# A second softplus whose 1 + u lives in PSUM, three bank pairs instead of four, and two smaller edits in a fused attention and feed-forward kernel

## What is computed

```python
scores = scale * q @ k_p.T            # attention over keys and values averaged by 8
x = softmax(scores) @ v_p             # -> x: 2304 tokens x 512
h = x @ w_in                          # first layer: 512 -> 2048
g = where(h >= 1, h, where(h <= -1, 0, (h + 1)**2 / 4))
x = g @ w_out                         # 2048 -> 512
h = x @ w2_in                         # second layer, the same sizes
g = maximum(h, 0) + log1p(exp(-abs(h)))
out = g @ w2_out
```

## Time and profile before

| | us |
|---|---|
| median of 3 runs | 862.84 |
| lowest and highest | 862.07 and 867.12 |
| the profiled execution | 862.46 |
| its span in the trace | 860.7 |

### The profile page before, as it was taken

The page is one execution under the profiler, slowest core; times in us unless marked ns, Lnnn a source line. Parts: engine busy times, 40 slices in busy tenths (PEclk is TensorE's granted clock), DMA queues, the critical chain, the costliest instruction groups (busy, mean ns, idle before and its releaser), DMA issues.

```text
span 860.7 us, 13035 instructions
## 1 busy us (share of the span) xinstructions
PE 845.8 (98%) x5198; PEld 822.7 (96%) x5198; DVE 592.0 (69%) x618; ACT 490.5 (57%) x700; POOL 360.8 (42%) x290
## 2 busy tenths in 40 slices
PE   8989999999999999999999999999999899999998
PEld 7768999999999999999999999999999899999998
DVE  4983855532233598768657698898899989778642
ACT  3875665644445453444435868978887654445442
POOL 6994677744454600000000498888766500000000
PEclk9979999999999999999999999999999999999999
DMA  8952767565555896454633235675655698645532
GB/s 195 209 126 78 209 209 230 185 220 188 181 183 188 274 395 224 167 220 154 227 109 99 96 123 189 211 243 182 211 200 176 204 397 306 239 164 203 200 113 73
DMA packets 106539, 167.82 MB, mean 195 GB/s; under 512 B 21872, under 2 KB 94448, under 8 KB 101872
## 3 DMA queue, kind: packets, MB, share of 16 engines
q1 hardware_dynamic: 93800, 157.86, 54.9%
q10 hardware_dynamic: 12680, 9.14, 3.7%
HBM read 96.21 MB, written 70.78 MB: 194 GB/s over the span
## 4 chain that ended last, share of the span: by engine, by line
PE 84%; DVE 6%; ACT 3%; DMA 3%; SPq 1%; issue 1%; POOL 1%; ACTq 0%; DVEq 0%
PE ps L1263 41%; PE ps L1281 37%; DVE t_a L1052 2%; DMA ops<-gops 2%; PE ps L1178 1%; DVE ops L1064 1%; PE ps L1215 1%; DMA w_raw<-in_moe_w_in_dram 1%; PE ps L1296 1%; PE ps L1321 1%; PE ps L1199 1%; DVE xs L992 1%; ACT qT L652 1%; PE ps L1155 1%; DVE t_a L1055 1%
## 5 line engine op out<-in xcount | busy, mean ns | idle before, releaser
L1263 PE MATMUL ps<-xs,W 128*128 128x384 f32 x2304 | 408.2, 336 | 0.8 <-DVE ops L1044 0.8
L1263 PEld LDWEIGHTS ps<-xs,W 128*128 128x128 f32 x2304 | 399.3, 188 | 5.8 <-issue 4.9
L1281 PE MATMUL ps<-xs,Tm 128*128 128x384 f32 x1968 | 345.9, 336 | 3.4 <-DVE xs L992 3.0
L1281 PEld LDWEIGHTS ps<-xs,Tm 128*128 128x128 f32 x1968 | 342.2, 189 | 4.3 <-issue 3.5
L744 ACT ACTIVATE xs<-ops 128x768 fp32r<-128x768 f32 (+1 forms) x148 | 111.7, 826 | 159.1 <-PE ps L1281 149.9
L608 POOL TENSOR_TENSOR ops<-ops 128x384 f32<-128x384 f32 x48 | 72.9, 1519 | 303.2 <-DVE ops L1064 221.9
L992 DVE TENSOR_TENSOR xs<-ops,xs 128x768 fp32r<-128x768 f32 (+1 forms) x148 | 130.2, 941 | 1.8 <-ACT xs L744 1.8
L1044 DVE SCALAR_TENSOR_TENSOR ops<-ps,t_a 128x768 f32<-128x768 f32 x48 | 45.9, 956 | 110.4 <-ACT t_a L768 110.2
L766 ACT ACTIVATE t_a<-ps 128x768 f32<-128x768 f32 x48 | 39.0, 812 | 96.2 <-PE ps L1263 96.2
L1077 DVE TENSOR_TENSOR X<-ps,X 128x768 f32<-128x768 f32 x41 | 38.7, 955 | 77.8 <-PE ps L1281 77.8
L1064 DVE TENSOR_TENSOR ops<-t_a,t_b 128x768 f32<-128x768 f32 x48 | 62.8, 1308 | 19.7 <-ACT t_b L787 17.9
(11 more groups left out here) (88 smaller groups left out, 650.6 us busy)
## 6 DMA issues: line engine op xcount, KB each, us to landing
gops<-ops SPq DMA_DIRECT2D x48, 1344.0 KB, 5.8
ops<-gops SPq DMA_DIRECT2D x36, 1536.0 KB, 6.8
X<-gops SPq DMA_DIRECT2D x22, 384.0 KB, 6.4
w_raw<-in_moe_w_in_dram SPq DMA_DIRECT2D x32, 256.0 KB, 3.9
t_raw<-in_moe_w_out_dram SPq DMA_DIRECT2D x6, 1024.0 KB, 10.0
out_dram<-y_out ACTq DMA_DIRECT2D x11, 384.0 KB, 2.6
k_raw<-in_k_dram SPq DMA_DIRECT2D x10, 288.0 KB
q_raw<-in_q_dram SPq DMA_DIRECT2D x20, 144.0 KB, 7.6
```

The costliest lines, as they stand in the source:

```text
L1263: last = mm(banks[:, tb, :], W[:, slot, f, part, c * P:(c + 1) * P], x[:, x_part, at:at + TB], start=c == 0 and s == 0, stop=c == KC - 1 a ...
L1281: last = mm(banks[:, d, :], Tm[:, t, part, j, d * P:(d + 1) * P], g[:, g_part, at * TB:(at + 1) * TB], start=at == 0 and s == 0, stop=at = ...
```

## The change

The softplus becomes: ScalarE |h| and u as before; b = 1 + u goes into the fourth pair of PSUM banks, of which there is one copy; l = ln b from there into one half of t_b. VectorE: s = max(h, 0) + u into the other half of t_b, as soon as u is there; e = (b - 1) - l, read from and written to the b banks; g = s - e. The sum is the same, in another order. Each b waits until the g of the pair before has been made, since that reads the b banks; s waits for the same g. ScalarE does the logarithm of a pair directly behind its 1 + u. The h pairs of the second layer go round three bank pairs, and line 1263 of pair a waits for s of pair a - 3. Step 3 of the second layer's products is the first to use the fourth pair again and waits for the last g.

The first product of each layer was copied to two blocks of X and is now copied to one; the addition that read the other copy reads this one. The hand-written places of fill 4 are gone from the second layer's end, which gets the plain order. SyncE issues the load of the fourth step's operand (fill 6) in quad 22 and no longer in quad 23, ahead of the store of quad 22.

```diff
-Y_OPS = (((0, 0, None), (0, 1, None)), ((0, 0, (0, 0)),), ((0, 1, (0, 1)),), ((1, 0, (0, 1)),),
+Y_OPS = (((0, 1, None),), ((0, 0, (0, 1)),), ((0, 1, (0, 1)),), ((1, 0, (0, 1)),),
+V_PAIRS, V_STEPS = HPAIRS + STEPS, 2 * HPAIRS + STEPS
+        def pair_of(v):
+            if v < SHARED:
+                return SHARED_BANKS[v % 2]
+            if v < V_PAIRS:
+                return ALL_BANKS[(v - SHARED) % 4]
+            if v < V_STEPS:
+                return ALL_BANKS[(V_PAIRS - SHARED + (v - V_PAIRS) % 3) % 4]
+            return ALL_BANKS[(V_PAIRS - SHARED + v - V_STEPS) % 4]
+        def b_banks():
+            b = 2 * ALL_BANKS[(V_PAIRS - SHARED + 3) % 4]
+            return ps[:, b:b + 2, 0:TB]
@@ banks_free
-            return spent[v - 2 if v < SHARED else v - 4]
+            if v == V_STEPS + 3:
+                return g_made, 2 * HPAIRS
+            if v < SHARED:
+                return spent[v - 2]
+            return spent[v - 3 if V_PAIRS + 3 <= v < V_STEPS + 3 else v - 4]
@@ sync
-                    if k == QUADS - 1:
+                    if k == QUADS - 2:
                         load_ops(layer, NT)
@@ scalar: plus_one, log
-                nc.scalar.activation(t_b[:, a % 2, :, :], t_a[:, a % 2, :, :], ACT.Copy, bias=1.0).then_inc(b_made, 1)
+                if a == 0:
+                    act.wait_ge(y_added, y_count(0, STEPS - 1))
+                else:
+                    act.wait_ge(g_made, HPAIRS + a)
+                nc.scalar.activation(b_banks(), t_a[:, a % 2, :, :], ACT.Copy, bias=1.0).then_inc(b_made, 1)
-                act.wait_ge(r_made, a + 1)
-                nc.scalar.activation(t_b[:, a % 2, :, :], t_b[:, a % 2, :, :], ACT.Ln).then_inc(l_made, 1)
+                act.wait_ge(b_made, a + 1)
+                nc.scalar.activation(t_b[:, 0, :, :], b_banks(), ACT.Ln).then_inc(l_made, 1)
@@ scalar: the loop
-                            if a == HPAIRS - 2:
-                                for piece in range(PIECES // 2):
-                                    fill_hi_piece(fill_of(1, NT + 1), piece)
                             exp_abs(a)
-                            if 0 < a < HPAIRS - 1:
-                                log(a - 1)
                             plus_one(a)
-                            if a == HPAIRS - 2:
-                                for piece in range(PIECES // 2, PIECES):
-                                    fill_hi_piece(fill_of(1, NT + 1), piece)
-                                log(a)
+                            log(a)
-                    if layer < m < STEPS:
+                    if m < STEPS:
@@ vector: softplus, total
-                u, b = t_a[:, a % 2, :, :], t_b[:, a % 2, :, :]
-                dve.wait_ge(b_made, a + 1)
-                nc.vector.scalar_tensor_tensor(out=u, in0=b, scalar=1.0, in1=u, op0=ALU.subtract, op1=ALU.subtract
-                                               ).then_inc(r_made, 1)
-                dve.wait_ge(r_made, a + 1)
-                nc.vector.scalar_tensor_tensor(out=u, in0=bank_pair(v_of_pair[n]), scalar=0.0, in1=u,
-                                               op0=ALU.max, op1=ALU.subtract).then_inc(s_made, 1)
+                if a:
+                    dve.wait_ge(g_made, HPAIRS + a)
+                dve.wait_ge(u_made, a + 1)
+                nc.vector.scalar_tensor_tensor(out=t_b[:, 1, :, :], in0=bank_pair(v_of_pair[HPAIRS + a]), scalar=0.0,
+                                               in1=t_a[:, a % 2, :, :], op0=ALU.max, op1=ALU.add).then_inc(s_made, 1)
+                dve.wait_ge(l_made, a + 1)
+                nc.vector.scalar_tensor_tensor(out=b_banks(), in0=b_banks(), scalar=1.0, in1=t_b[:, 0, :, :],
+                                               op0=ALU.subtract, op1=ALU.subtract).then_inc(e_made, 1)
                 dve.wait_ge(s_made, a + 1)
-                dve.wait_ge(l_made, a + 1)
+                dve.wait_ge(e_made, a + 1)
                 dve.wait_ge(*slot_free(u))
-                nc.vector.tensor_tensor(g, t_a[:, a % 2, :, :], t_b[:, a % 2, :, :], ALU.add).then_inc(g_made, 1)
+                nc.vector.tensor_tensor(g, t_b[:, 1, :, :], b_banks(), ALU.subtract).then_inc(g_made, 1)
@@ vector: the loop
                             softplus(a)
-                            if a == HPAIRS - 3:
-                                for piece in range(PIECES // 2):
-                                    fill_lo_piece(fill_of(1, NT + 1), piece)
                             total(a)
-                            if a == HPAIRS - 2:
-                                for piece in range(PIECES // 2, PIECES):
-                                    fill_lo_piece(fill_of(1, NT + 1), piece)
-                    if layer < m < STEPS:
+                    if m < STEPS:
```

More of the change, by code:

```diff
@@ L222, in build @@
         h_abs, u_made, b_made = sem("h_abs"), sem("u_made"), sem("b_made")
-        r_made, s_made, l_made = sem("r_made"), sem("s_made"), sem("l_made")
+        s_made, l_made, e_made = sem("s_made"), sem("l_made"), sem("e_made")
         g_made, s_added = sem("g_made"), sem("s_added")
@@ L247, in wait @@
                 eng.wait_ge(semaphore, value)
+        def pair_of(v):
[6 more added lines that the diff above has]
+            return ALL_BANKS[(V_PAIRS - SHARED + v - V_STEPS) % 4]
         def bank_pair(v):
-            b = 2 * (SHARED_BANKS[v % 2] if v < SHARED else ALL_BANKS[(v - SHARED) % 4])
+            b = 2 * pair_of(v)
+            return ps[:, b:b + 2, 0:TB]
+        def b_banks():
+            b = 2 * ALL_BANKS[(V_PAIRS - SHARED + 3) % 4]
             return ps[:, b:b + 2, 0:TB]
@@ L870, in _ @@
                         fill_hi_piece(fill_of(layer, NT), k - FIRST_AT)
-                if layer == 1:
-                    log(HPAIRS - 1)
                 for m in range(1, STEPS + 2):
-                    if layer < m < STEPS:
+                    if m < STEPS:
                         for piece in range(PIECES):
@@ L1047, in softplus @@
             def softplus(a):
-                n = HPAIRS + a
-                u, b = t_a[:, a % 2, :, :], t_b[:, a % 2, :, :]
-                dve.wait_ge(b_made, a + 1)
-                nc.vector.scalar_tensor_tensor(out=u, in0=b, scalar=1.0, in1=u, op0=ALU.subtract, op1=ALU.subtract
-                                               ).then_inc(r_made, 1)
-                dve.wait_ge(r_made, a + 1)
-                nc.vector.scalar_tensor_tensor(out=u, in0=bank_pair(v_of_pair[n]), scalar=0.0, in1=u,
-                                               op0=ALU.max, op1=ALU.subtract).then_inc(s_made, 1)
+                if a:
[3 more added lines that the diff above has]
+                                               in1=t_a[:, a % 2, :, :], op0=ALU.max, op1=ALU.add).then_inc(s_made, 1)
             def total(a):
                 u, g = g_of(HPAIRS + a)
+                dve.wait_ge(l_made, a + 1)
+                nc.vector.scalar_tensor_tensor(out=b_banks(), in0=b_banks(), scalar=1.0, in1=t_b[:, 0, :, :],
+                                               op0=ALU.subtract, op1=ALU.subtract).then_inc(e_made, 1)
                 dve.wait_ge(s_made, a + 1)
-                dve.wait_ge(l_made, a + 1)
+                dve.wait_ge(e_made, a + 1)
                 dve.wait_ge(*slot_free(u))
-                nc.vector.tensor_tensor(g, t_a[:, a % 2, :, :], t_b[:, a % 2, :, :], ALU.add).then_inc(g_made, 1)
+                nc.vector.tensor_tensor(g, t_b[:, 1, :, :], b_banks(), ALU.subtract).then_inc(g_made, 1)
             def add_y(layer, m):
```

## The result

| | before | after |
|---|---|---|
| median of 20 runs, us | 865.93 | 861.21 |
| lowest | 862.0 | 856.38 |
| profiled execution | 862.46 | 857.14 |
| its span | 860.7 | 855.3 |

The ratio of the runs after to the runs before is **0.994, with a 95% interval from 0.992 to 0.996** (a few runs of each kernel that lie far above the others are left out): 0.6% faster, less than the 1% that the prediction took as the border of "the same". The forecast for the profiled execution was 857.3, and it took 857.14; 862.84 x 0.994 is 857.7, the forecast of the median.

What follows compares the result with a forecast made beforehand. TensorE, with work 98% of the span, was taken as the bound, losing 5.7 us behind the second h stage. 47.40 becomes 41.70 + 0.4 + 0.1 = 42.2, 5.2 us less: 857.3 profiled, median 857.7 us, range 855.8 to 867.

Steps and rivals of the forecast that it cites:

- one verdict: Whole kernel: within 1% of before, chance 0.89; faster by over 1% 0.02, slower by over 1% 0.09.
- The loss before: End of the second h stage through the fifth step: 47.40 us where 41.70 are needed, 5.7 us lost.
- The cause: Second h stage: VectorE's two operations with both inputs in SBUF are blocked by GpSimd's sums, 3.80 us a pair.
- The unknown cost of writing PSUM: Three instructions using b in PSUM: excess zero; bounds 0.1 us less each and, above, one stream doubled, 0.96 to 1.76.
- The ring: Second-layer softplus, serial through the one b buffer (1 + u, ln, e, g, next 1 + u): 3.81 us against TensorE's 4.17.
- The lag of pair 44: Quad 21 of the second h stage: VectorE's weights push s of pair 44 to 6.96 us after its matmuls.
- the last g: End of the second h stage: g of pair 47 done 7.76 us after the last pair's matmuls end.
- The rival's price: Second h stage, softplus chain becomes the bound: full doubling 883 us, chance over 871 0.09; middle 862 to 870, 0.11 shared.
- break-even of 0.3 us: Softplus chain through b: an excess of 0.3 us a pair would eat the 5.7 us of gain.
- rival (2): End of the second h stage stays late by another cause, smaller gain: 858.9 to 862.5 us, chance 0.20.
- Three pairs: Second-layer h pairs on three bank pairs: 5.5 us in reserve, so TensorE shouldn't wait in the h stage.
- The plain order: Fill 4 behind the second h stage: new wait of 0.3 to 0.5 us before the second step; 2.05 us wait goes.

Runs made afterwards that it cites:

- experiment 4: Kernel before with GpSimd's four sums per second-layer quad cut to 8 of 384 columns; ratio to before 0.9912; second h stage's start to first output transpose 241.29 us.
- experiment 6: Changed kernel with the single b buffer in SBUF in place of PSUM, all else as changed; ratio to the kernel before 1.0146.
- experiment 5: Kernel before, old softplus kept, with only its second-layer h pairs going round three bank pairs; ratio to the kernel before 1.0117.
- experiment 3: Changed kernel with the first product copied twice and the load of fill 6 in quad 23 again; ratio to the kernel before 0.9922.
- experiment 8: Changed kernel with 1 + u of each pair done twice over all columns, one behind the other; ratio to the kernel before 1.0279.
- experiment 2: Kernel before with its old softplus and all the other edits of the change; ratio to the kernel before 1.0003.
- experiment 7: Changed kernel with 1 + u of 16 of the 768 columns first and the full one behind a wait for it; ratio to the kernel before 0.9945.

## Why the prediction was right

**What the time alone says.** Little: the range of 855.8 to 867 also holds the 862.84 of no change, and 0.89 of the chances stood on one verdict. The forecast is tested by the places and terms below.

**The loss before.** 5.7 us were counted behind the stage and 5.2 of them forecast as won; 5.6 were won in S to M, of 6.05 that experiment 4's 241.29 leaves to win. The cause, blocked two-input SBUF operations, was argued from three rows; experiment 4 shows it by taking the sums away, and experiment 6 by putting b back into SBUF.

**The unknown cost of writing PSUM.** I took an excess of zero from the nearest rows; it was 0.01 us on VectorE and below zero on ScalarE. With the surcharge for a PSUM source that the Trainium skill's table gives ("VectorE: DVE Perf Modes", the TRN2 errata) the ring would be 3.94 us, an estimate from that table, and the verdict the same. It measured 3.80. The step from e to g did come out 0.07 longer than forecast (1.06), but with b in SBUF it is 1.05 (experiment 6, 630.27 to 631.32), so the trace doesn't show the surcharge.

**The ring.** 3.81 forecast, 3.80 measured. That the sum is right to 0.01 is partly luck: ln to e was 0.07 shorter and e to g 0.07 longer than the distances that I had taken from the old softplus. The lag of pair 44 was 6.7 for 6.96, the last g T + 7.5 for T + 7.76, both 0.3 us earlier than forecast. The rival's price was right where it was tried: 0.85 us more give 1.0279, where the prediction's rule (0.49 x 48 and 5 at the end, less 5.7, that is 22.8 us) gives 1.026. Its break-even of 0.3 us was not tried; at 0.2 the kernel is still 4.3 us faster than before from S to M, where rival (2) expected a gain of 1 to 2 us: the wait was 1.49 us and not 2.4, and no low clock came.

**Three pairs.** They are enough, as forecast, but this was the term that I understood least: experiment 5's 8.7 us against the 4 to 6 expected show how fast a lag turns into waits once cover is short.

**The plain order.** Its new wait was forecast at 0.3 to 0.5 us. The profile shows 0.17 idle behind the modelled end of the first step, and 0.34 more than 48 matmuls from that step's start to the next (668.34 to 677.00), so the size is right. The edit is worth 1.5 us with the new softplus and costs 2.3 us with the old (with the two small edits beside it).

**Copies and load.** Costed at nothing, worth nothing (experiment 3).

**The time itself.** 857.7 was right as a ratio. As a number it was tied to the median of three runs; the twenty runs put both kernels 3 to 4 us higher.

## What to carry to other kernels

Where GpSimd and VectorE both work on SBUF, look for VectorE instructions whose mean is far above their minimum, and move one of their two inputs to PSUM: three instructions for three, and 3.8 us a pair became 2.9. Before a serial ring through one buffer is accepted, add its four start-to-start distances from the trace and hold them against the pace of the bounding engine; 0.36 us of room was enough here; a ring 0.34 us too long on average (experiment 6) or 0.49 us too long (experiment 8) cost all the gain and more. A hand-written order serves one set of durations: when they change, try the plain one again.

## What the runs showed that I had not expected

**Where the scatter comes from.** The second h stage begins at 468.36 us in the profile of before and at 476.97 in that of experiment 2, though the two programs are the same up to 300 us. Pieces of the two chains in order of time, first before, then experiment 2:

```profile
17.90 1.24 PE ps L1178 x20
...
189.60 104.20 PE ps L1263 x600
```

```profile
17.61 2.14 PE ps L1165 x20
...
25.30 1.24 PE ps L1165 x20
...
198.21 104.20 PE ps L1250 x600
```

The third group of this kind starts 7.4 us later in experiment 2 (25.30 against 17.90), the 600 matmuls 8.6 us later. So most of the difference arises in the first 25 us, where 20 matmuls that take 1.24 us elsewhere take 2.14 (17.61), nearly twice as long. Two windows of experiment 2:

```profile
10.00:20.00 10.00, 10.00 (x67) 9.51 (x68) 2.99 (x6) 1.95 (x5) 8.03 (x9) 1.00 0.96 214
60.00:65.00 5.00, 5.00 (x35) 3.91 (x35) 2.77 (x7) 3.16 (x8) 3.77 (x4) 0.50 1.06 223
```

The view prints a clock of 1.00 for the first window. At 61.65 us, where it prints 0.50, the same group of 20 takes 2.21 us again. So it was probably the low clock at the start as well, and the view does not show it; that is inferred from the durations. In all ten profiles the second h stage begins 278.8 us behind the start of the 600 matmuls, whatever the variant, and that start lies anywhere from 189.5 to 198.1 us. A difference of a few us between two profiles of this kernel thus says nothing unless it is counted from S on. Of the twenty runs after, the seven with a mean clock of 0.984 to 0.988 took 861.5 to 864.2 us, the four with 0.994 to 0.996 took 856.4 to 858.0, which fits this.

**A wait and the clock.** After a wait the clock did not always fall, and the length of the wait alone doesn't tell when. Behind 1.41 and 1.66 us (experiment 6) and 1.49 us (experiment 7) it stayed at 1.00. Behind 2.05 us (before), 2.42 (experiment 6), 2.43 and 3.19 (experiment 8) and 4.95 (experiment 2) TensorE ran at 0.50 for a while, which cost 1.5 to 2.2 us. But in experiment 5 the clock stayed at 1.00 behind waits of 2.17 and 2.35 us and fell behind one of 2.40, and in experiment 8 it stayed behind one of 2.40 (682.03). Experiment 5, behind 2.35 and behind 2.40 us:

```profile
676.00:680.20 4.20, 4.20 (x24) 4.20 (x25) 3.41 (x3) 0.44 (x1) 0.77 (x1) 1.00 0.62 219
709.10:713.00 3.90, 3.90 (x14) 3.90 (x15) 3.90 (x4) 1.07 (x2) 0.00 (x0) 0.59 0.99 378
```

So a wait of 2.05 to 2.4 us was paid nearly twice in some places and once in others; what decides it these runs leave open.
